# The second sequence's last two transforms over even and odd rows apart, and two waits of TensorE for its own last product, in a Fourier transform with two layers behind it

## The chip, the cores and the metric

The kernel runs on one core of a Trainium2 chip. The metric is the device time of one execution in microseconds; the profile gives the span from the first to the last instruction and every instruction's start and duration. The engines are TensorE (PE; its weight loads are listed apart as PEld), VectorE (DVE), ScalarE (ACT), GpSimd (POOL) and SyncE (SP), which issues most DMAs.

## The reference

```python
batch, seq, dim = (2, 3008, 256)        # x; d_ff = 2048
def _attn_ref(x):
    X = np.fft.fft(x, axis=1)
    X = np.fft.fft(X, axis=2)
    return X.real.astype(np.float32)
def _moe_ref(x, w_in, w_out):
    h = x @ w_in
    g = h * (1.0 / (1.0 + np.exp(-h)))
    return (g @ w_out).astype(np.float32)
def _moe2_ref(x, w_in, w_out, alpha):
    h = x @ w_in
    g = np.maximum(h, 0.0) + alpha * np.minimum(h, 0.0)
    return (g @ w_out).astype(np.float32)
# x -> _attn_ref -> reshape(6016, 256) -> _moe_ref -> _moe2_ref
```

The real part of a two-dimensional Fourier transform of two sequences is followed by two layers of 256 to 2048 to 256 features over all 6016 tokens.

## The kernel before, in words

**Transforms.** The feature transform is folded into the first layer's weights (`ab`). The transform over 3008 positions is folded by symmetry to 377 rows, held in three tiles of 128 (even rows in the first 192 places, odd rows in the last 192), and done with cosine tables for four blocks of output positions (`BLOCK_K`). Blocks 0 and 1 ("t1") already work on even and odd rows apart: one sum over the even rows (E), one over the odd rows (O), and the two blocks are E + O and E - O. Blocks 2 and 3 ("t2", "t3") are each one product over all three tiles, 376 or 378 columns wide, for each of the two halves p and q of the features (`transform23`, L571). These products are in float32, which TensorE does in two passes; the trace has a record for each pass. Everything else is split into high and low parts, and a product is three matmuls in fp32r of one pass each (`three`, L363 to L365).

**First layer.** It runs in `STEPS1` = 96 steps g: six chunks of 502 tokens by 16 slices of 128 hidden features. In step g TensorE does `first1(g)` (6 matmuls) and `second1(g - 2)` (12 matmuls, L626, L627 and L630). Between them ACT copies v out of PSUM (L927), DVE makes h in three operations (L1218, L1221, L1223), ACT makes the activation twice (L860 into `gh`, L863 into `g_sb`), and POOL subtracts them to `gl` (L1388), for which the last four matmuls of the step, L630, wait (`gl_done`).

**Turns.** The first sequence's transforms run before the steps. Those of the second run as jobs after certain steps (`JOB_AFTER`). A step or a job is a turn, and turns alternate between two pairs of PSUM banks; `turn_free` makes a turn wait until the turn before the last was read out. So while jobs stand between steps, each step waits for the h of the step just before it.

**The row of middle features.** Row 0 of the operands belongs to the middle feature. For block 3 of the second sequence it is made early, kept in `n_hold`, and written over row 0 of `pq` once the last t3 transform has been split: `n_hold_round` on ACT and `n_hold_low` on DVE (L1174), in step 38. SP waits for that (`t23_lo` at its full count), stores the rows of chunks 3 to 5 to DRAM (`store_n`, L437), waits for it, and loads chunk 3's row back over all partitions (`load_n(3)`, L431). POOL adds the two parts of what was loaded (`add_n`, L1326): `add_n(3)` stands behind `gl` of step 40, and POOL takes its work in program order:

```python
                if f == NF // 2 and c + 1 < NC1:
                    add_n(c + 1)
```

with `c, f = divmod(g, 16)`, and in it `pool.wait_ge(n_in, 16 * c)`.

**Second layer.** It has 48 units of 7 products of 3 matmuls (a fast scheme with seven products for eight, `products_a` and `products_b`) and 24 matmuls of `second2` (L684, L685, L688). Its weights are prepared by POOL and ACT during the steps from `W_STEP` on.

Of the kernel before, what the change touches and what calls it, by code (L numbers as in the profile page):

```python
# [7 lines left out]
F32 = mybir.dt.float32  # L8
# [4 lines left out]
P = 128  # L13
# [3 lines left out]
S2, S4, S8 = S // 2, S // 4, S // 8  # L17
QT = -(-(S8 + 1) // P)
NT = QT * BATCH
BLOCK_K = [list(range(1, S2, 4)), [S2 - k for k in range(1, S2, 4)], list(range(2, S2, 4)), list(range(0, S2 + 1, 4))]  # L20
BLOCK_W = [len(k) + len(k) % 2 for k in BLOCK_K]
BLOCK_AT = [sum(BLOCK_W[:i]) for i in range(4)]
COLS = sum(BLOCK_W)
# [15 lines left out]
A_JOBS = [(1, 0), (0, 0), (1, 1), (0, 1), (1, 2), (0, 2), (1, 3), (0, 3)]  # L39
FOLD_AFTER = [*range(3, 16, 2), *range(18, 32)]  # L40
IDLE = 4
JOB_AFTER = {1: "n", 33: "t1p", 34: "t1q", 35: "t2", 36: "t3"}


def cut(at, width):
# [20 lines left out]
def build(nc, x_tiles, x_half, moe_w_in, moe_w_out, moe2_w_in, moe2_w_out, alpha_cols, feat_dft, two_eye, t1, t2, t3, out_t):  # L66
    ctx = ExitStack()
    with ctx:
# [190 lines left out]
        def item_view(i):  # L259
# [5 lines left out]

        T_JOBS = [(1, 0, "p"), (1, 0, "q"), (2, 0, "p"), (2, 0, "q"), (3, 0, "p"), (3, 0, "q"), (3, None, "n"),
                  (1, 1, "p"), (1, 1, "q"), (2, 1, "p"), (2, 1, "q"), (3, 1, "p"), (3, 1, "q")]
        T1_JOBS = [j for j in T_JOBS if j[0] == 1]

        T23_JOBS = [j for j in T_JOBS if j[0] > 1] + ["n_hold"]  # L270

# [12 lines left out]
        def t1_of(*job):  # L284
            return T1_JOBS.index(job) + 1

        def t23_of(*job):
            return T23_JOBS.index(job) + 1
# [8 lines left out]
        def pair_at(turn):  # L297
            return 2 * (TURNS.index(turn) % 2)
# [6 lines left out]
        def t_bank(blk, b, s):  # L305

            if s == "n":
                return pair_at("n") + blk - 2
            if b == 0:
                return {1: 1, 2: 4, 3: 6}[blk] + (2 if blk == 1 else 1) * (s == "q")  # L310
            if blk == 1:
                return pair_at("t1" + s) + 1
            return pair_at(f"t{blk}") + (s == "q")

        def e_bank(b, s):
            return t_bank(1, b, s) - 1

        A2_BANK, N0_BANK = 7, 2

        def turn_free(pe, turn):  # L320

            i = TURNS.index(turn)
            if i < 2:
                pe.wait_ge(t1_sum, i + 1)
                pe.wait_ge(o_done, i + 1)
                return
            former = TURNS[i - 2]
            if former == "n":
                pe.wait_ge(t23_lo, t23_of(3, None, "n"))
            elif former in ("t1p", "t1q"):  # L330
                pe.wait_ge(t1_sum, t1_of(1, 1, former[2]))
                pe.wait_ge(o_done, t1_of(1, 1, former[2]))
            elif former in ("t2", "t3"):
                pe.wait_ge(t23_lo, t23_of(int(former[1]), 1, "q"))
            else:
                pe.wait_ge(h_done, former + 1)

# [5 lines left out]
                eng.wait_ge(mm1, STEPS1)  # L343


        W_STEP = [41, 57]
        W_SUMS = {"s1": ("a21", "a22"), "s3": ("a11", "a21"), "s2": ("s1", "a11"), "s4": ("a12", "s2")}
        W_STAGE = ["a11", "a12", "a22", "a21"]
        W_HI_AT = {"a11": 0, "a12": 0, "a22": 1, "s1": 2, "s3": 3, "s2": 4, "s4": 5}
# [42 lines left out]
        def _(sp):  # L392
# [77 lines left out]
            sp.wait_ge(stage_lo, WO2_ITEM)  # L470
            load_w7(0)
            store_x1(0)
            sp.wait_ge(t1_lo, len(T1_JOBS))
            sp.wait_ge(t1_late, len(T1_JOBS))
            sp.wait_ge(t23_lo, len(T23_JOBS))
            store_n(NC1 // 2, NC1)
            sp.wait_ge(n_out, 64)
# [37 lines left out]
        def _(pe):  # L515
# [45 lines left out]
            def transform23(blk, b, s, qs=range(QT)):  # L561

                sb, w = (t2_sb, BLOCK_W[2]) if blk == 2 else (t3_sb, BLOCK_W[3])
                half = 1 if s == "q" else 0
                dst = ps[0:72 if s == "n" else P, t_bank(blk, b, s), 0:w]
                for q in qs:
                    if s == "n":
                        st = nop[:, q:q + 72]
                    else:
                        st = op_b[QT * b + q][:, {2: (3, 0), 3: (1, 2)}[blk][half], :]  # L570
                    ins = pe.matmul(dst, st, sb[:, q, half * w:(half + 1) * w], start=q == 0, stop=q == QT - 1)  # L571
                if q == QT - 1:
                    ins.then_inc(t_pe, 1)

            def job(name):

                turn_free(pe, name)
                if name == "n":
                    pe.wait_ge(nop_ready, BATCH)
                    transform23(3, None, "n")  # L580
                elif name in ("t1p", "t1q"):
                    pe.wait_ge(fold, fold_at(NT - 1) + 7)
                    for blk in range(2):
                        for q in (blk, blk + 1):
                            transform1(1, name[2], blk, q)
                else:
                    pe.wait_ge(fold, fold_at(NT - 1) + FOLDS)
                    for s in "pq":
                        transform23(int(name[1]), 1, s)

            def first1(g):

# [133 lines left out]
            transform23(3, 0, "q")  # L726
            job(JOB_AFTER[LAG - 1])
            for g in range(LAG, STEPS1):
                first1(g)
                second1(g - LAG)  # L730
                if g in JOB_AFTER:
                    job(JOB_AFTER[g])
# [3 lines left out]
            second1(STEPS1 - 1)  # L736
            for u in range(1, UNITS):
                products_a(u)
                second2(u - 1, 0)
                second2(u - 1, 1)  # L740
                products_b(u)
                second2(u - 1, 2)
                second2(u - 1, 3)
# [5 lines left out]
        def _(act):  # L749
# [26 lines left out]
                act.wait_ge(fold, fold_rest_at(t) + 1)  # L776
                act.copy(op_b[t][:, 0, 0:1], nfold3[:, 3, NT + t:NT + t + 1]).then_inc(middle_in, 1)

            def t1_copy(b, s):

                act.wait_ge(t_pe, t_pe_of(1, b, s))
                if b:
                    act.wait_ge(t1_sum, 2)
                O = ps[:, t_bank(1, b, s), 0:T1W]
                if s == "q":
                    act.activation(o_sb[:, 2, :], O, ACT.Identity, scale=n_sign[:, 0:1])
                act.copy(o_sb[:, "pq".index(s), :], O).then_inc(o_done, 1)

            def t1_round(b, s):

# [11 lines left out]
            def t23_round(blk, b, s):  # L802

                act.wait_ge(t_pe, t_pe_of(blk, b, s))
                bank = t_bank(blk, b, s)
                if s == "n":
                    act.wait_ge(t23_lo, t23_of(blk, 0, "q"))
                    act.copy(n_hold[0:1, 0:BLOCK_W[blk]], ps[32:33, bank, 0:BLOCK_W[blk]])
                for c, o, a, w in cut(BLOCK_AT[blk], BLOCK_W[blk]):
                    if s == "n":  # L810
                        ins = act.copy(pq[0:1, c, 2, o:o + w], ps[0:1, bank, a:a + w])
                    else:
                        ins = act.copy(pq[:, 3 * b + c, 2 * (s == "q"), o:o + w], ps[:, bank, a:a + w])
                ins.then_inc(t23_hi, 1)

            def n_hold_round():
# [117 lines left out]
            for g in range(1, STEPS1):  # L934
                if g >= 2:
                    silu_high(g - 1)
                    copy_v(g)
                    silu_whole(g - 1)
                if g % NF == LAG - 1 and g >= NF:
                    store_x1_minus(g // NF - 1)  # L940
                if g == 1:
                    t23_round(3, 0, "p")
                    t23_round(3, 0, "q")
                turn = JOB_AFTER.get(g)
                if turn == "n":
                    t23_round(3, None, "n")
                elif turn in ("t1p", "t1q"):
                    t1_copy(1, turn[2])
                elif turn in ("t2", "t3"):
                    t23_round(int(turn[1]), 1, "p")  # L950
                    t23_round(int(turn[1]), 1, "q")
                former = JOB_AFTER.get(g - 1)
                if former in ("t1p", "t1q"):
                    t1_round(1, former[2])
                    t1_late_round(1, former[2])
                elif former == "t3":
                    n_hold_round()
                if 2 <= g <= 2 * WO2_ITEM - 4 and g % 2 == 0:
                    split_hi(g // 2 + 1)
                for q, at0 in enumerate(W_STEP):  # L960
                    for w, k in W_HI_AT.items():
                        if g == at0 + k:
                            w7_round(q, w)
                if g in X_STEP_HI:
                    xr_round(0, X_STEP_HI.index(g))
# [38 lines left out]
        def _(dve):  # L1004
# [124 lines left out]
            def t1_sums(b, s):  # L1129
# [9 lines left out]
                                                (ALU.add, ALU.subtract)[blk])  # L1139
                ins.then_inc(t1_sum, 1)  # L1140

            def t1_low(b, s):

                dve.wait_ge(t1_hi, t1_of(1, b, s))
                for blk, a, w, hi, raw, lo in t1_pieces(b, s, 0):
                    ins = dve.tensor_tensor(lo, raw, hi.bitcast(F32), ALU.subtract)
                ins.then_inc(t1_lo, 1)
# [62 lines left out]
            for g in range(STEPS1):  # L1210
# [23 lines left out]
                if turn == "n":  # L1234
                    t23_low(3, None, "n")
                elif turn in ("t1p", "t1q"):
                    t1_sums(1, turn[2])
                elif turn in ("t2", "t3"):
                    t23_low(int(turn[1]), 1, "p")
                    t23_low(int(turn[1]), 1, "q")  # L1240
                former = JOB_AFTER.get(g - 2)
                if former in ("t1p", "t1q"):
                    t1_low(1, former[2])
                    t1_late_low(1, former[2])
                elif former == "t3":
                    n_hold_low()
                if g in FOLD_AFTER:
                    i = FOLD_AFTER.index(g)
# [292 lines left out]
```

## Time and profile before

| what | value |
|---|---|
| median of 3 runs | 948.46 us |
| the three runs | 934.04, 948.46 and 949.15 us |
| the profiled execution | 928.23 us |
| its span, and mean granted clock | 926.3 us, 0.999 |
| PE, PEld busy | 920.9 us, 757.8 us |
| DVE, ACT, POOL busy | 625.9, 561.3 and 573.4 us |

Busy time of PE is modelled and overlaps from one matmul to the next (a matmul of 502 columns is listed with 385 ns, and the next starts 0.22 us after it), so pace is read from starts, not from durations.

### The profile page before, as it was taken

How to read it: one execution, taken by the hardware profiler on the slowest of the kernel's cores; microseconds unless marked ns; L12 is line 12 of the kernel's file. 1: busy time of each engine (PE TensorE's matmuls, PEld its weight loads, DVE VectorE, ACT ScalarE, POOL GpSimd, SP SyncE). 2: the span in 40 equal slices, each digit the busy share in tenths (PEclk: the TensorE clock that was granted, in tenths of full speed). 3: DMA queues.
4: the chain of work that ended last, by engine and by line, in shares of the span. 5: the costliest groups of instructions: out<-in, count | busy, mean ns of one | idle time of the engine just before them, and what ended most of it. 6: DMA issues, size and time to landing. Idle time of an engine off the chain costs nothing.

```text
span 926.3 us, 11845 instructions
## 1 busy us (share of the span) xinstructions
PE 920.9 (99%) x4034; PEld 757.8 (82%) x4034; DVE 625.9 (68%) x964; ACT 561.3 (61%) x873; POOL 573.4 (62%) x408
## 2 busy tenths in 40 slices
PE   9999999999999999999999999999999999999998
PEld 4688888778888888888888888888888888888886
DVE  5877799464544544544877777787787777777774
ACT  4677666557668666676765555565555555555554
POOL 0477655337877867676697477566647756764443
PEclk9999999999999999999999999999999999999999
DMA  9510200002110220100400200020020002001001
GB/s 354 231 56 24 90 1 1 1 1 90 45 46 23 70 66 1 45 1 1 136 1 1 90 1 1 1 89 1 1 90 1 0 1 90 1 1 44 1 1 45
DMA packets 19825, 40.35 MB, mean 44 GB/s; under 512 B 1802, under 2 KB 15668, under 8 KB 18740
## 3 DMA queue, kind: packets, MB, share of 16 engines
q1 hardware_dynamic: 18980, 39.05, 12.0%
q8 instruction: 32, 0.52, 0.2%
q10 hardware_dynamic: 688, 0.52, 0.2%
q14 instruction: 29, 0.24, 0.1%
q0 software_dynamic: 96, 0.02, 0.0%
HBM read 27.22 MB, written 12.37 MB: 43 GB/s over the span
## 4 chain that ended last, share of the span: by engine, by line
PE 99%; ACT 0%; DVE 0%; issue 0%
PE ps L363 13%; PE ps L365 13%; PE ps L364 13%; PE ps L626 9%; PE ps L630 9%; PE ps L627 9%; PE ps L688 9%; PE ps L684 9%; PE ps L685 9%; PE ps L571 2%; PE ps L527 2%; PE ps L556 1%; PE ps L552 1%; PE ps L694 0%; PE ps L543 0%; ACT out_sb L998 0%
## 5 line engine op out<-in xcount | busy, mean ns | idle before, releaser
L1410 POOL TENSOR_TENSOR gl<-g,gh 128x502 fp32r<-128x502 f32 x192 | 224.8, 1177 | 173.4 <-ACT gh L906 173.3
L1388 POOL TENSOR_TENSOR gl<-g_sb,gh 128x1004 fp32r<-128x1004 f32 x96 | 207.9, 2165 | 134.2 <-ACT g_sb L863 133.8
L900 ACT ACTIVATE g<-ps 128x502 f32<-128x502 f32 x192 | 112.0, 592 | 109.8 <-DVE ps L1267 104.9
L1218 DVE SCALAR_TENSOR_TENSOR h_sb<-n_all,a,ps 128x502 f32<-128x502 f32 x96 | 70.7, 736 | 140.9 <-ACT v_sb L927 140.6
L860 ACT ACTIVATE gh<-h_sb 128x1004 fp32r<-128x1004 f32 x96 | 100.6, 1048 | 90.1 <-DVE h_sb L1223 90.1
L1274 DVE SCALAR_TENSOR_TENSOR g<-g,less_alpha,ps 128x502 f32<-128x502 f32 x192 | 132.7, 732 | 32.7 <-ACT g L900 32.7
L626 PE MATMUL ps<-gh,wo 128*128 128x502 f32 x384 | 148.6, 387 | 0.0
L627 PE MATMUL ps<-gh,wo 128*128 128x502 f32 x384 | 147.4, 384 | 0.0
L685 PE MATMUL ps<-gh,wo 128*128 128x502 f32 x382 | 147.2, 385 | 0.0
L684 PE MATMUL ps<-gh,wo 128*128 128x502 f32 x382 | 147.2, 385 | 0.0
L906 ACT CAST gh<-g 128x502 fp32r<-128x502 f32 x192 | 113.0, 614 | 40.3 <-DVE g L1274 38.6
L688 PE MATMUL ps<-gl,wo 128*128 128x502 f32 x382 | 116.3, 385 | 0.0
L1267 DVE TENSOR_TENSOR ps<-ps,h 128x502 f32<-128x502 f32 x144 | 98.1, 689 | 5.0
L630 PE MATMUL ps<-gl,wo 128*128 128x502 f32 x384 | 101.4, 385 | 0.0
L863 ACT ACTIVATE g_sb<-h_sb 128x1004 f32<-128x1004 f32 x96 | 100.7, 1049 | 0.0
L626 PEld LDWEIGHTS ps<-gh,wo 128*128 128x128 f32 x384 | 72.0, 187 | 14.4
L630 PEld LDWEIGHTS ps<-gl,wo 128*128 128x128 f32 x384 | 72.0, 188 | 13.7
L688 PEld LDWEIGHTS ps<-gl,wo 128*128 128x128 f32 x382 | 71.7, 188 | 13.7
L684 PEld LDWEIGHTS ps<-gh,wo 128*128 128x128 f32 x382 | 71.7, 188 | 13.6
L685 PEld LDWEIGHTS ps<-gh,wo 128*128 128x128 f32 x382 | 71.7, 188 | 13.6
L627 PEld LDWEIGHTS ps<-gh,wo 128*128 128x128 f32 x384 | 72.1, 188 | 13.1
L363 PE MATMUL ps<-pq,ab 128*128 128x502 f32 x192 | 75.9, 396 | 0.0
(137 smaller groups left out, 1583.0 us busy)
## 6 DMA issues: line engine op xcount, KB each, us to landing
x_tile<-x_tiles SPq DMA_DIRECT2D x6, 1024.0 KB, 13.4
x_rows<-x SPq DMA_DIRECT2D x6, 1004.0 KB, 5.9
out_t<-out_sb SPq DMA_DIRECT2D x11, 502.0 KB, 3.2
x_raw_b<-x_rows SPq DMA_DIRECT2D x18, 251.0 KB, 4.2
stage<-moe_w_out SPq DMA_DIRECT2D x16, 256.0 KB, 4.1
n_parts<-n_rows SPq DMA_DIRECT2D x5, 502.0 KB, 3.5
stage<-moe_w_in SPq DMA_DIRECT2D x8, 256.0 KB, 3.5
w_sb<-moe_w_in SPq DMA_DIRECT2D x3, 512.0 KB, 8.7
```

The source lines that it names most:

```text
L363: pe.matmul(dst, sh, mh, start=first, stop=False)
L364: pe.matmul(dst, sh, ml, start=False, stop=False)
L365: return pe.matmul(dst, sl, mh, start=False, stop=last)
L626: pe.matmul(dst, wh, gh[g % 2][:, sg, :], start=f == 0, stop=False)
L627: pe.matmul(dst, wl, gh[g % 2][:, sg, :], start=False, stop=False)
L630: ins = pe.matmul(dst, wo1[:, f, 0, ft * P:(ft + 1) * P], gl[g % 2][:, sg, :], start=False, stop=f == NF - 1)
L684: pe.matmul(out[ft], wh, gh4[:, k, :], start=fp == 0 and k < 2, stop=False)
L685: pe.matmul(out[ft], wl, gh4[:, k, :], start=False, stop=False)
L688: ins = pe.matmul(out[ft], wo2[:, f, 0, ft * P:(ft + 1) * P], gl4[:, k, :], start=False, stop=fp == HF - 1 and k >= 2)
L1274: dve.scalar_tensor_tensor(out=g4[:, k, :], in0=g4[:, k, :], scalar=less_alpha[:, f:f + 1], in1=product_bank(u, TILE_IN[k]), op0=ALU.mult, ...
L1388: pool.tensor_tensor(gl[g % 2][:, :, :], g_sb[g % 2][:, :, :], gh[g % 2][:, :, :].bitcast(F32), ALU.subtract).then_inc(gl_done, 1)
L1410: pool.tensor_tensor(gl4[:, k, :], g4[:, k, :], gh4[:, k, :].bitcast(F32), ALU.subtract).then_inc(gl_done, 1)
```

## The change

The columns of blocks 2 and 3 are put in another order: first the positions k up to a quarter of the sequence, then their mirror images. For the mirror image of k the even rows count alike and the odd rows with the other sign, so `transform23_parted` makes E and O with half the columns (188 or 189) each, from four matmuls of 128, 64, 64 and 128 rows. ACT copies O to SBUF, DVE makes E + O and E - O, ACT rounds them and DVE makes the low parts (`t23_sums`, `t23_parted_round`, `t23_parted_low`). Each half p and q is now a turn by itself, so there are six jobs instead of four, after steps 32 to 37. The work on `n_hold` stands three and four steps behind the last job, where it stood one and two steps behind; in steps that is 40 (ACT) and 41 (DVE). The second layer's weights are prepared two steps later. TensorE waits for the end of `second1(0)` ahead of `first1(3)`, and for the end of its last product ahead of the first `second2` of the second unit.

```diff
-BLOCK_K = [list(range(1, S2, 4)), [S2 - k for k in range(1, S2, 4)], list(range(2, S2, 4)), list(range(0, S2 + 1, 4))]
+BLOCK_K = [list(range(1, S2, 4)), [S2 - k for k in range(1, S2, 4)], [*range(2, S4, 4), *(S2 - k for k in range(2, S4, 4))],
+           [*range(0, S4 + 1, 4), *(S2 - k for k in range(0, S4, 4))]]
...
-JOB_AFTER = {1: "n", 33: "t1p", 34: "t1q", 35: "t2", 36: "t3"}
+JOB_AFTER = {1: "n", 32: "t1p", 33: "t1q", 34: "t2p", 35: "t2q", 36: "t3p", 37: "t3q"}
...
-        W_STEP = [41, 57]
+        W_STEP = [43, 59]
...
+            def transform23_parted(blk, s):
+
+
+                sb, w = (t2_sb, BLOCK_W[2]) if blk == 2 else (t3_sb, BLOCK_W[3])
+                half, h = w * (s == "q"), w // 2
+                m = {2: (3, 0), 3: (1, 2)}[blk][s == "q"]
+                for o, parts in ((0, ((0, 0, P), (1, 0, P // 2))), (1, ((1, P // 2, P), (2, 0, P)))):
+                    dst = ps[:, e_bank(1, s, blk) + o, 0:h]
+                    for i, (q, r0, r1) in enumerate(parts):
+                        ins = pe.matmul(dst, op_b[QT + q][r0:r1, m, :], sb[r0:r1, q, half:half + h],
+                                        start=i == 0, stop=i == 1)
+                ins.then_inc(t_pe, 1)
...
-                    for s in "pq":
-                        transform23(int(name[1]), 1, s)
+                    transform23_parted(int(name[1]), name[2])
...
+                if g == LAG + 1:
+                    pe.wait_ge(mm2, 1)
                 first1(g)
...
                 products_a(u)
+
+                if u == 1:
+                    pe.wait_ge(prod_a, 8)
                 second2(u - 1, 0)
...
-                elif former == "t3":
+                elif former != "n":
+                    t23_parted_round(int(former[1]), former[2])
+                if JOB_AFTER.get(g - 3) == "t3q":
                     n_hold_round()
...
+            def t23_sums(blk, s):
+
+
+                dve.wait_ge(o_done, t1_of(blk, 1, s))
+                h, m = BLOCK_W[blk] // 2, 2 * (s == "q") + 1
+                for half in range(2):
+                    for c, o, a, w in cut(BLOCK_AT[blk] + half * h, h):
+                        E, O = ps[:, e_bank(1, s, blk), a:a + w], o_sb[:, "pq".index(s), a:a + w]
...
-                elif former == "t3":
+                elif former != "n":
+                    t23_parted_low(int(former[1]), former[2])
+                if JOB_AFTER.get(g - 4) == "t3q":
                     n_hold_low()
```

The first place is TensorE at the last transform job, with the end of `second1` ahead of it and the first matmul of the next step behind it; before:

```order
L630 MATMUL ps<-gl_92,wo_83 128x502 [waits gl_done]
L630 MATMUL ps<-gl_92,wo_83 128x502 x3
L571 MATMUL ps<-t_sb,op_b_58 128x378 [waits fold,t23_lo]
L571 MATMUL ps<-t_sb,op_b_59 128x378
L571 MATMUL ps<-t_sb,op_b_60 128x378
L571 MATMUL ps<-t_sb,op_b_58 128x378
L571 MATMUL ps<-t_sb,op_b_59 128x378
L571 MATMUL ps<-t_sb,op_b_60 128x378
L363 MATMUL ps<-pq,ab 128x502 [waits h_done]
```

And with the change, on the same engine at the same place:

```order
L641 MATMUL ps<-gl_93,wo_83 128x502 [waits gl_done]
L641 MATMUL ps<-gl_93,wo_83 128x502 x3
L583 MATMUL ps<-t_sb,op_b_58 128x189 [waits fold,o_done,t1_sum]
L583 MATMUL ps<-t_sb,op_b_59 128x189 x2
L583 MATMUL ps<-t_sb,op_b_60 128x189
L362 MATMUL ps<-pq,ab 128x502 [waits h_done]
```

A job of six matmuls of 378 columns has become two of four matmuls of 189 columns, with a step between them; the two in the middle, on `op_b_59`, take 64 rows each.

The second place is DVE from step 37 on: three operations L1218, L1221 and L1223 are the h of one step, and L1174 is the low part of the `n_hold` row, on which SP waits. Before, two steps' h and then it:

```order
L1218 SCALAR_TENSOR_TENSOR h_sb_79<-n_all_76,a_162,ps 128x502 [waits silu_done,v_done]
L1221 TENSOR_TENSOR h_sb_79<-ps,v_sb 128x502
L1223 TENSOR_TENSOR h_sb_79<-ps,h_sb_79 128x502 [waits w_done]
L1218 SCALAR_TENSOR_TENSOR h_sb_78<-n_all_76,a_162,ps 128x502 [waits silu_done,v_done]
L1221 TENSOR_TENSOR h_sb_78<-ps,v_sb 128x502
L1223 TENSOR_TENSOR h_sb_78<-ps,h_sb_78 128x502 [waits w_done]
L1174 TENSOR_TENSOR pq<-n_hold,pq 1x378 [waits t23_hi]
```

With the change the same row is L1221; ahead of it stand the last low parts of t3 (L1185, in steps 38 and 39) and the h of steps 39 to 41 (L1265, L1268 and L1270):

```order
L1185 TENSOR_TENSOR pq<-pq_raw,pq 128x378 [waits t23_hi]
L1265 SCALAR_TENSOR_TENSOR h_sb_79<-n_all_76,a_162,ps 128x502 [waits silu_done,v_done]
L1268 TENSOR_TENSOR h_sb_79<-ps,v_sb 128x502
L1270 TENSOR_TENSOR h_sb_79<-ps,h_sb_79 128x502 [waits w_done]
L1185 TENSOR_TENSOR pq<-pq_raw,pq 128x378 [waits t23_hi]
L1265 SCALAR_TENSOR_TENSOR h_sb_78<-n_all_76,a_162,ps 128x502 [waits silu_done,v_done]
L1268 TENSOR_TENSOR h_sb_78<-ps,v_sb 128x502
L1270 TENSOR_TENSOR h_sb_78<-ps,h_sb_78 128x502 [waits w_done]
L1265 SCALAR_TENSOR_TENSOR h_sb_79<-n_all_76,a_162,ps 128x502 [waits silu_done,v_done]
L1268 TENSOR_TENSOR h_sb_79<-ps,v_sb 128x502
L1270 TENSOR_TENSOR h_sb_79<-ps,h_sb_79 128x502 [waits w_done]
L1221 TENSOR_TENSOR pq<-n_hold,pq 1x378 [waits t23_hi]
```

The row has moved from step 38 to step 41.

The third place is POOL at step 40: L1388 is `gl` of one step, L1326 is `add_n(3)`, L1340 the first work on the second layer's weights. Before:

```order
L1388 TENSOR_TENSOR gl_92<-g_sb_81,gh_90 128x2x502 [waits silu_done,gh_done]
L1326 TENSOR_TENSOR n_all_76<-n_parts 128x502 [waits w_done,n_in]
L1388 TENSOR_TENSOR gl_93<-g_sb_82,gh_91 128x2x502 [waits silu_done,gh_done]
L1340 TENSOR_TENSOR w_raw_s_109<-stage_158,stage_157 128x512 [waits stage_in3,t_pe,stage_in2,t23_lo,stage_in1,stage_in0]
L1388 TENSOR_TENSOR gl_92<-g_sb_81,gh_90 128x2x502 [waits silu_done,gh_done]
```

With the change (`gl` is L1436, `add_n` L1374 and the weights L1388):

```order
L1436 TENSOR_TENSOR gl_92<-g_sb_81,gh_90 128x2x502 [waits silu_done,gh_done]
L1374 TENSOR_TENSOR n_all_76<-n_parts 128x502 [waits w_done,n_in]
L1436 TENSOR_TENSOR gl_93<-g_sb_82,gh_91 128x2x502 [waits silu_done,gh_done]
L1436 TENSOR_TENSOR gl_92<-g_sb_81,gh_90 128x2x502 [waits silu_done,gh_done]
L1436 TENSOR_TENSOR gl_93<-g_sb_82,gh_91 128x2x502 [waits silu_done,gh_done]
L1388 TENSOR_TENSOR w_raw_s_109<-stage_158,stage_157 128x512 [waits stage_in3,t_pe,stage_in2,t23_lo,stage_in1,stage_in0]
```

The work on the weights has moved back by two steps; `add_n(3)` stands where it stood, behind `gl` of step 40.

## Rows read from the trace of the kernel before

**Rows 1.** The page's first part: busy time, share, instructions.

```profile
PE 920.9 (99%) x4034; PEld 757.8 (82%) x4034; DVE 625.9 (68%) x964; ACT 561.3 (61%) x873; POOL 573.4 (62%) x408
```

**Rows 2.** The waits of PE, whole run: total, times, longest (us).

```profile
PE ps L694 <- DVE pq_raw L1178: 1.2, 1, 1.2
```

**Rows 3.** The chain that ended last, steps 35 to 38: start, length (us), what.

```profile
184.55 0.89 PE ps L630 x4
185.44 3.79 PE ps L571 x12
...
192.37 0.89 PE ps L630 x4
193.26 3.81 PE ps L571 x12
...
200.21 0.89 PE ps L630 x4
...
204.23 0.89 PE ps L630 x4
```

**Rows 4.** The timeline of PEld (weight loads), around a product of one row.

```profile
33.79 0.19 PEld L365 LDWEIGHTS ps<-pq,ab 128*128 128x128 f32 x1
34.33 0.29 PEld L543 LDWEIGHTS ps<-pq,ones 1*128 1x128 f32 x2 [0.36 <-issue]
34.98 0.19 PEld L363 LDWEIGHTS ps<-pq,ab 128*128 128x128 f32 x1 [0.36 <-issue]
35.09 0.19 PEld L364 LDWEIGHTS ps<-pq,ab 128*128 128x128 f32 x1
```

**Rows 5.** The timeline of PE at the same place.

```profile
34.01 0.39 PE L365 MATMUL ps<-pq,ab 128*128 128x502 f32 x1
34.33 0.72 PE L543 MATMUL ps<-pq,ones 1*128 1x502 f32 x2
```

**Rows 6.** The timeline of PE, in steps 36 and 38.

```profile
190.19 0.39 PE L365 MATMUL ps<-pq,ab 128*128 128x502 f32 x1
...
202.06 0.39 PE L365 MATMUL ps<-pq,ab 128*128 128x502 f32 x1
...
204.06 1.06 PE L630 MATMUL ps<-gl,wo 128*128 128x502 f32 x4
```

**Rows 7.** The timeline of ACT: v copied out, with a job and without one.

```profile
191.54 0.57 ACT L927 COPY v_sb<-ps 128x502 f32<-128x502 f32 x1
...
202.48 0.58 ACT L927 COPY v_sb<-ps 128x502 f32<-128x502 f32 x1 [0.24 <-PE ps L365]
```

**Rows 8.** The timeline of DVE: the last third of h, and the `n_hold` row.

```profile
193.40 0.67 DVE L1223 TENSOR_TENSOR h_sb<-ps,h_sb 128x502 f32<-128x502 f32 x1
...
204.34 0.67 DVE L1223 TENSOR_TENSOR h_sb<-ps,h_sb 128x502 f32<-128x502 f32 x1
204.92 1.79 DVE L1174 TENSOR_TENSOR pq<-n_hold,pq 1x378 fp32r<-1x378 f32 x1
```

**Rows 9.** The timeline of SP's queue after it.

```profile
206.80 1.39 SPq L437 DMA_DIRECT2D n_rows<-pq  x2
209.41 0.33 SPq L431 DMA_DIRECT2D n_parts<-n_rows  x1
```

**Rows 10.** L431's own view, its five loads.

```profile
DMA to landing us min/median/max: 3.4/3.5/4.2
```

**Rows 11.** The timeline of POOL, `gl` of steps 40 and 41.

```profile
216.21 2.16 POOL L1388 TENSOR_TENSOR gl<-g_sb,gh 128x1004 fp32r<-128x1004 f32 x1 [1.85 <-ACT g_sb L863]
218.32 1.08 POOL L1326 TENSOR_TENSOR n_all<-n_parts 128x502 f32<-128x502 f32 x1
220.22 2.17 POOL L1388 TENSOR_TENSOR gl<-g_sb,gh 128x1004 fp32r<-128x1004 f32 x1 [0.82 <-ACT g_sb L863]
```

**Rows 12.** Stretches: start:end, length, PE busy to POOL busy, granted clock, DMA.

```profile
450.00:900.00 450.00, 450.00 (x2017) 378.02 (x2016) 335.59 (x499) 253.64 (x449) 284.06 (x241) 1.00 0.08 27
922.40:926.30 3.90, 0.00 (x0) 0.00 (x0) 0.00 (x0) 0.26 (x1) 0.00 (x0) 0.88 0.70 264
```

More of the change, by code:

```diff
@@ L267, in build @@
                   (1, 1, "p"), (1, 1, "q"), (2, 1, "p"), (2, 1, "q"), (3, 1, "p"), (3, 1, "q")]
-        T1_JOBS = [j for j in T_JOBS if j[0] == 1]
+        T1_JOBS = [j for j in T_JOBS if j[0] == 1 or j[1] == 1]
         T23_JOBS = [j for j in T_JOBS if j[0] > 1] + ["n_hold"]
@@ L310, in t_bank, with e_bank @@
                 return {1: 1, 2: 4, 3: 6}[blk] + (2 if blk == 1 else 1) * (s == "q")
[L311 to L316, printed above, removed]
+            return pair_at(f"t{blk}{s}") + 1
+        def e_bank(b, s, blk=1):
+            return t_bank(blk, b, s) - 1
         A2_BANK, N0_BANK = 7, 2
@@ L329, in turn_free @@
                 pe.wait_ge(t23_lo, t23_of(3, None, "n"))
[L330 to L334, printed above, removed]
+            elif isinstance(former, str):
+                pe.wait_ge(t1_sum, t1_of(int(former[1]), 1, former[2]))
+                pe.wait_ge(o_done, t1_of(int(former[1]), 1, former[2]))
             else:
@@ L472, in _ @@
             store_x1(0)
[L473 to L474 removed]
+            sp.wait_ge(t1_lo, 2 * BATCH)
+            sp.wait_ge(t1_late, 2 * BATCH)
             sp.wait_ge(t23_lo, len(T23_JOBS))
@@ L777, in middle2, with t1_copy @@
                 act.copy(op_b[t][:, 0, 0:1], nfold3[:, 3, NT + t:NT + t + 1]).then_inc(middle_in, 1)
-            def t1_copy(b, s):
-                act.wait_ge(t_pe, t_pe_of(1, b, s))
+            def t1_copy(b, s, blk=1):
+                act.wait_ge(t_pe, t_pe_of(blk, b, s))
                 if b:
-                    act.wait_ge(t1_sum, 2)
-                O = ps[:, t_bank(1, b, s), 0:T1W]
-                if s == "q":
+                    act.wait_ge(t1_sum, t1_of(blk, b, s) - 2)
+                w = BLOCK_W[blk] // (1 if blk == 1 else 2)
+                O = ps[:, t_bank(blk, b, s), 0:w]
+                if s == "q" and blk == 1:
                     act.activation(o_sb[:, 2, :], O, ACT.Identity, scale=n_sign[:, 0:1])
-                act.copy(o_sb[:, "pq".index(s), :], O).then_inc(o_done, 1)
+                act.copy(o_sb[:, "pq".index(s), 0:w], O).then_inc(o_done, 1)
             def t1_round(b, s):
@@ L813, in t23_round, with t23_parted_round @@
                         ins = act.copy(pq[:, 3 * b + c, 2 * (s == "q"), o:o + w], ps[:, bank, a:a + w])
+                ins.then_inc(t23_hi, 1)
+            def t23_parted_round(blk, s):
+                act.wait_ge(t1_sum, t1_of(blk, 1, s))
+                for c, o, a, w in cut(BLOCK_AT[blk], BLOCK_W[blk]):
+                    m = 2 * (s == "q")
+                    ins = act.copy(pq[:, 3 + c, m, o:o + w], pq_raw[:, 3 + c, m + 1, o:o + w])
                 ins.then_inc(t23_hi, 1)
@@ L946, in _ @@
                     t23_round(3, None, "n")
[L947 to L952, printed above, removed]
+                elif turn:
+                    t1_copy(1, turn[2], int(turn[1]))
+                former = JOB_AFTER.get(g - 1, "n")
                 if former in ("t1p", "t1q"):
@@ L1140, in t1_sums, with t23_parted_low @@
                 ins.then_inc(t1_sum, 1)
+            def t23_sums(blk, s):
[4 more added lines that the diff above has]
+                        E, O = ps[:, e_bank(1, s, blk), a:a + w], o_sb[:, "pq".index(s), a:a + w]
+                        if half and (blk, s) == (3, "q"):
+                            E, O = O, E
+                        ins = dve.tensor_tensor(pq_raw[:, 3 + c, m, o:o + w], E, O, (ALU.add, ALU.subtract)[half])
+                ins.then_inc(t1_sum, 1)
+            def t23_parted_low(blk, s):
+                dve.wait_ge(t23_hi, t23_of(blk, 1, s))
+                for c, o, a, w in cut(BLOCK_AT[blk], BLOCK_W[blk]):
+                    m = 2 * (s == "q")
+                    ins = dve.tensor_tensor(pq[:, 3 + c, m + 1, o:o + w], pq_raw[:, 3 + c, m + 1, o:o + w],
+                                            pq[:, 3 + c, m, o:o + w].bitcast(F32), ALU.subtract)
+                ins.then_inc(t23_lo, 1)
             def t1_low(b, s):
@@ L1237, in _ @@
                     t1_sums(1, turn[2])
[L1238 to L1241, printed above, removed]
+                elif turn:
+                    t23_sums(int(turn[1]), turn[2])
+                former = JOB_AFTER.get(g - 2, "n")
                 if former in ("t1p", "t1q"):
```

## The prediction

> **What bounds the kernel now.** Read the page's first part and then the waits. PE is busy for 99% of the span and no other engine for more than 68% [rows 1]; in the whole run PE is listed as waiting once, 1.2 us at the very start [rows 2]. The chain that ended last is PE from one end to the other, so its places tell what a step costs: from one group of L630 to the next without a job 4.02 us (200.21 to 204.23), for 18 matmuls, 223.3 ns each; with a transform job in between 7.82 us (184.55 to 192.37) [rows 3]. So the kernel is a string of 3888 matmuls of 502 columns (96 steps of 18, 48 units of 45; 868 us) with the transforms and the start around it. Only two sorts of edit can move the end: work taken out of that string, and a gap put into it. Anything on DVE, ACT, POOL or a queue counts only when it comes late for PE.
>
> **The level of a run.** The profiled execution took 928.23 us, its span 926.3, so 1.9 us lie around it. The three timed ones took 934.04, 948.46 and 949.15. The trace shows no place where 20 us could be found but the string itself: 20.2 us over 3888 matmuls is 5.2 ns each, 228.5 ns instead of 223.3. I make the sum against 928.23 and treat the level as a question of its own below.
>
> **Part 1, the transforms.** Before, each of two jobs is 12 passes of 376 or 378 columns in 3.79 and 3.81 us, 316 ns a pass, 7.6 us together [rows 3]. After, four turns have 8 passes each of 188 or 189 columns. 316 ns is 378 columns at 0.84 ns; by that, a pass of 188 takes 158 ns, a turn 1.27 us, four 5.1 us. But the middle matmuls use 64 rows. The nearest thing in the trace is L543, a product over one row: its weight load is not made ahead but starts 0.32 us after L365's start, at 34.33, and weight loads stand 0.11 us apart (34.98 and 35.09), so its product starts near 34.44, 0.43 us behind L365 instead of 0.22 [rows 4, 5]; on the way back the load of L363 stands at 34.98, again 0.32 us behind the second L543. A change between whole and partial rows so costs 0.21 us, and a turn has two: 1.7 us, four 6.8 us, a gain of **0.8 us**. Ends: two such changes and a third between the halves, 1.9 us a turn, no gain; none, and the two halves beside each other, 0.95 us a turn, gain 3.8. I take 0.8, as the rows of L543 are the same event.
>
> The Trainium skill, "TensorE: Matmul & The Clock Gate" (Part 3), says that matmuls on different row groups run at the same time; the halves stand on rows 0 to 63 and 64 to 127, and by it the sum would be up to 1.3 us lower. No row here shows two such products side by side, so it moves only my lower end.
>
> **Part 2, turns that share a pair of banks.** From step 33 to 38 each step needs the h of the step just before. In step 36 of before, with ACT busy with earlier rounds, h was done (193.40 + 0.67) 3.9 us after v's last product started at 190.19; v's copy began only at 191.54, while without jobs it begins 0.42 us after that product's start (202.06, 202.48) [rows 6 to 8]. After, PE has 0.22 + 12 x 0.223 + 1.3 to 1.9, so 4.2 to 4.8 us of its own work there. The cover holds by 0.3 us or more: **0**, upper end 1.5 us if ACT's additional rounds delay v by another 0.6 us in five steps.
>
> **Part 3, the row in n_hold.** This is the term that I put most on. DVE's L1174 moves from step 38 to step 41, and behind it hang SP's store, SP's load and, on POOL, `add_n(3)`, which stays in step 40 with everything that POOL has to do queued behind it. In the times of before: L1174 starts at 204.92 and ends at 206.71 [rows 8]; SP issues the store at 206.80 and, when that has landed, the load at 209.41 [rows 9]; it lands 3.4 to 4.2 us later [rows 10], at 213.6 at the latest. POOL asks for it at 218.32, so 4.7 us are to spare [rows 11]. Three steps later, 12.06 us: L1174 ends at 218.77, the load is issued at 221.47 and lands at 225.7 (4.2 us; I take the long one, as a 1 MB store is issued right behind it). POOL stands from 218.4 to 225.7. Then L1326 takes 1.08 and `gl` of step 41 2.17 us: done at 228.9, where before it ended at 222.39 [rows 11]. PE asks for it with L630 at 204.06 + 5 x 4.02 = 224.16 [rows 3, 6]. With 0.1 us for the weight load [rows 4] L630 starts at 229.1: a gap of **4.9 us** in the string. Then POOL, with 2.17 us of `gl` in a step of 4.02 and the weights' work put back two steps, has caught up a step later, so it is paid once. Lower end 2.9: landing after 3.4 us, and L1174 in 0.6 instead of 1.79 us (a like third of h takes 0.67 over 128 rows [rows 8]). Upper end 5.5, a store slower by 0.6. The threshold is plain: up to 7.2 us of delay are free (4.7 of the landing, the 0.82 that POOL idles ahead of `gl` at 220.22, 1.8 between `gl` and L630), and 12.06 are asked for.
>
> **Part 4, PE's waits for its own last product.** A product's result is taken by another engine when its listed 0.39 us are over plus 0.03 (202.06, 202.48) [rows 6, 7]; then come semaphore and weight load, 0.11 [rows 4]: 0.53 us from start to start in place of 0.22, so **0.3 us** each, 0.6 together. Ends: 0.21, as for L543, and 0.45 if the load's whole 0.19 us has to pass. Queued behind each wait is PE's own string; the others lose nothing, since their idle time is larger in every step (ACT waits 0.24 us for v alone in a step without a job [rows 7]).
>
> **The sum.** 928.23 - 0.8 + 0 + 4.9 + 0.6 = 932.9 us; with all lower ends 928.23 - 3.8 + 2.9 + 0.4 = 927.7, with all upper ends 928.23 + 0 + 1.5 + 5.5 + 0.9 = 936.1.
>
> **Rivals.**
>
> *The string stays at the slow level.* If timed runs of the changed kernel keep the 228.5 ns a matmul that 948.46 implies, the gap is added to the median instead: 948.46 + 4.7 = 953 us, slower than before. It turns on the pace: above 227.3 ns a matmul the changed kernel is above 948.46. For it: two of three runs stood there, nothing in the profile says what sets it, and steps 2 to 95 pass six jobs that restart the string anyway, as before. Against it: both new waits empty PE at the start of each stage, and the gap of part 3 restarts it once more; if the level is a matter of how the string starts, they can set it. 0.3.
>
> *The gap isn't there* (the row is not late, because SP's chain is quicker than in the trace, or POOL's order differs from what is built): 928.23 - 0.8 + 0.6 = 928.0 us. It needs the chain of 6.9 us (206.71 to 213.6) to shrink to 2.0. 0.08 with the low level.
>
> *The transforms gain nothing and the turns stall:* 936 us, in the range of my forecast.
>
> *The clock falls in the gap.* Behind the last matmul the granted clock of the last 3.9 us is 0.88 [rows 12], which at 1.0 and 0.5 means that it fell from 2.4 to 1.2 GHz some 3 us after PE stopped. A gap of 4.9 us is longer. If it falls in the gap and stays low for a time as long as it took to fall, 3 us of matmuls take double: 1.5 us more, 934.5 us. 0.25 of all, inside the range. "TensorE: Matmul & The Clock Gate" of the Trainium skill (Part 1) names the same two levels and says that idleness brings the lower one; the trace agrees by the 0.88.
>
> *The waits themselves bring a pace quicker than 223.3.* No row shows one: the steps of the first stage stand 4.02 us apart [rows 3], and 450 us of the second hold 2017 matmuls [rows 12], 223.1 ns each. 0.02.
>
> **How the numbers follow.** Low level with the gap (clock steady or not): 0.55, 928 to 936, forecast **933 us**. High level: 0.33 (with the gap 0.3), around 953. No gap, low level: 0.08. Others 0.04. Both signs hold much, so the likeliest case's own range is 929 to 937; the range to be given must reach into the high level: **928 to 954**. Against the median of 948.46, 2% is about what a measurement of this kernel can tell from no change; faster by over 2% is below 929.5: the case without the gap, the low end of the forecast (mostly the transforms at their best), and a before that is measured higher: 0.17. Slower by over 2% needs the high level against a before that comes out near 934: 0.08. Within 2%: 0.75.
>
> **What would show it.** Right: on PE a wait on POOL's `gl` (L641) of 4 to 5 us in step 43, once, and on POOL `n_all` (L1374) waiting 7 us for the DMA of `n_parts`; L583 in four groups of 8 passes, 1.7 us each with weight loads not ahead in the middle; gaps of 0.3 us at the first L362 of step 3 and the first L695 of the second unit; no wait of PE between steps 32 and 38. Wrong: no wait of PE on POOL, or one that comes again in later steps; the L583 groups under 1.3 or over 1.9 us; above all, a pace other than 223.3 ns in the windows of the two stages, or timed runs that scatter as those of before did.

## The result, and the profile after

The changed kernel took 934.06 us, the median of 22 runs (932.76 to 935.58). The kernel before, run beside it 22 times, took 931.94 us (927.66 to 949.78). The ratio is 1.0044 with a 95% interval of 1.003 to 1.0058, for which the runs of before at 948 us and more are left out: the change costs 0.4%, and against the ten runs of before at 928 us alone (median 927.94) 0.7%. With all 22 runs in, the mean of before is 935.9 us and that of the changed kernel 934.0, so what the change costs depends on how often a run of before stands high. The forecast of 933 us was met within 1.1 us as a time; as a step from the median shown then (948.46) it had the wrong sign. Seven of the 22 runs of before stood at 948 to 950 us, four near 934 and the others mostly near 928; of the changed kernel none left its 3 us. That is a second effect of the change, and half of the experiments are about it.

The profiled execution took 933.65 us with a span of 931.8, 5.5 us more than before. PE's waits in the changed kernel (total, times, longest), to read beside [rows 2]:

```profile
PE ps L641 <- POOL gl L1436: 4.6, 1, 4.6
PE ps L705 <- DVE pq_raw L1225: 1.2, 1, 1.2
PE ps L526 <- DMA mt<-feat_dft: 0.5, 1, 0.5
```

The first line is new, and it is a single wait; the third, new too, is for a load at the start. The timeline of POOL shows what was ahead of it, to read beside [rows 11]:

```profile
214.84 2.17 POOL L1436 TENSOR_TENSOR gl<-g_sb,gh 128x1004 fp32r<-128x1004 f32 x1 [1.85 <-ACT g_sb L889]
224.33 1.07 POOL L1374 TENSOR_TENSOR n_all<-n_parts 128x502 f32<-128x502 f32 x1 [7.32 <-DMA n_parts<-n_rows]
225.36 4.25 POOL L1436 TENSOR_TENSOR gl<-g_sb,gh 128x1004 fp32r<-128x1004 f32 x2
```

POOL stands idle for 7.32 us until the row of chunk 3 has landed; then come `add_n(3)` and two `gl` in a row. DVE's `n_hold` row and SP's queue behind it, beside [rows 8, 9]:

```profile
215.63 1.78 DVE L1221 TENSOR_TENSOR pq<-n_hold,pq 1x378 fp32r<-1x378 f32 x1
```

```profile
217.50 1.39 SPq L436 DMA_DIRECT2D n_rows<-pq  x2
220.10 0.33 SPq L430 DMA_DIRECT2D n_parts<-n_rows  x1
```

From the row's end at 217.41 to the load's issue are 2.69 us, and 4.2 more to POOL's start at 224.33: the same chain as before, begun three steps later. PE at the gap, its timeline:

```profile
222.58 0.39 PE L638 MATMUL ps<-gh,wo 128*128 128x502 f32 x1
227.55 1.47 PE L641 MATMUL ps<-gl,wo 128*128 128x502 f32 x4 [4.57 <-POOL gl L1436]
228.82 0.62 PE L362 MATMUL ps<-pq,ab 128*128 128x502 f32 x1
229.24 0.62 PE L363 MATMUL ps<-pq,ab 128*128 128x502 f32 x1
```

From 222.58 to 227.55 are 4.97 us in place of 0.22. And then the matmuls of the next step start 0.42 us apart, not 0.22. The stretches around it (length, busy of PE, PEld, DVE, ACT, POOL, granted clock, DMA):

```profile
224.00:226.00 2.00, 0.00 (x0) 0.00 (x0) 0.00 (x0) 0.00 (x0) 1.67 (x2) 1.00 0.92 345
226.00:228.00 2.00, 0.45 (x2) 0.41 (x3) 0.00 (x0) 0.00 (x0) 2.00 (x2) 1.00 0.68 147
228.00:229.00 1.00, 1.00 (x5) 0.78 (x4) 0.00 (x0) 0.00 (x0) 1.00 (x1) 0.63 0.66 237
229.00:230.00 1.00, 1.00 (x4) 0.81 (x3) 0.00 (x0) 0.89 (x1) 0.62 (x1) 0.50 0.03 12
230.00:231.00 1.00, 1.00 (x4) 0.76 (x3) 0.00 (x0) 0.15 (x1) 0.00 (x0) 0.50 0.00 0
231.00:232.00 1.00, 1.00 (x5) 0.81 (x4) 0.00 (x0) 0.43 (x1) 0.00 (x0) 0.66 0.00 0
```

By the shares of these stretches the granted clock is 0.50 from about 228.3 to 231.7: 1.2 in place of 2.4 GHz. PE had been empty for 4.6 us and was running again for 0.7 us when it fell. Eight matmuls take 0.2 us more each, 1.6 us. The Trainium skill's "TensorE: Matmul & The Clock Gate" (Part 1) has idleness bring this level, and the trace agrees: the fall comes behind the only long gap.

The chain at the last four turns, beside [rows 3]:

```profile
181.15 0.89 PE ps L641 x4
182.04 1.35 PE ps L583 x8
186.71 0.89 PE ps L641 x4
187.60 1.35 PE ps L583 x8
192.09 0.89 PE ps L641 x4
192.99 1.36 PE ps L583 x8
197.48 0.89 PE ps L641 x4
198.37 1.36 PE ps L583 x8
202.87 0.89 PE ps L641 x4
```

The steps are 5.56, 5.38, 5.39 and 5.39 us, against 4.02 without a job: four turns cost 5.6 us in place of 7.6, a gain of 2.0. The weight loads of the first turn:

```profile
181.66 0.41 PEld L583 LDWEIGHTS ps<-t_sb,op_b 128*128 128x128 f32 x2
182.29 0.30 PEld L583 LDWEIGHTS ps<-t_sb,op_b 64*128 64x128 f32 x4 [0.22 <-issue]
182.81 0.30 PEld L583 LDWEIGHTS ps<-t_sb,op_b 128*128 128x128 f32 x2 [0.22 <-issue]
183.31 0.19 PEld L362 LDWEIGHTS ps<-pq,ab 128*128 128x128 f32 x1 [0.20 <-DVE h_sb L1270]
```

Four loads of 64 rows fit into 0.30 us, where two of 128 take 0.30 too: lower and upper half are loaded side by side. The loads that aren't made ahead, by 0.22 us at each change of mode, are there as well. The last row is a wait for h, 0.2 us, once.

The two waits for its own product, the timeline of PE:

```profile
44.42 1.05 PE L641 MATMUL ps<-gl,wo 128*128 128x502 f32 x4
45.54 0.49 PE L362 MATMUL ps<-pq,ab 128*128 128x502 f32 x1
45.87 0.39 PE L363 MATMUL ps<-pq,ab 128*128 128x502 f32 x1
...
451.74 0.38 PE L364 MATMUL ps<-x_t,w_s 128*128 128x502 f32 x1
452.18 0.49 PE L695 MATMUL ps<-gh,wo 128*128 128x502 f32 x1
452.51 0.39 PE L696 MATMUL ps<-gh,wo 128*128 128x502 f32 x1
```

At each, two starts are 0.44 and 0.33 us apart instead of twice 0.22 (451.74, 452.18, 452.51): 0.33 us, two 0.65. PE also comes to step 2 later than before: its L641 stands at 44.42, before L630 stood at 44.12, 0.3 us that the transforms and the waits have no part in. The wait for h is in the 5.6 us of the turns. So the sum of what the trace shows is -2.0 + 4.75 + 1.6 + 0.65 + 0.3 = 5.3 of the 5.5 us.

### The profile page after: what moved, and what is told of

It reads as the page before. It is cut to its first block, busy times and chain, and to the rows that moved or that the text cites. A ratio compares the mean times of both kernels' runs of the same rounds, so it can differ in the third digit from the quotient of the medians.

```text
span 931.8 us, 11884 instructions
## 1 busy us (share of the span) xinstructions
PE 921.0 (99%) x4042; PEld 757.4 (81%) x4042; DVE 630.9 (68%) x974; ACT 562.1 (60%) x877; POOL 573.7 (62%) x408
## 4 chain that ended last, share of the span: by engine, by line
PE 98%; issue 1%; POOL 0%; DMA 0%; ACT 0%; POOLq 0%
PE ps L362 13%; PE ps L364 13%; PE ps L363 13%; PE ps L695 9%; PE ps L696 9%; PE ps L699 9%; PE ps L641 9%; PE ps L637 9%; PE ps L638 9%; PE ps L526 2%; PE ps L555 1%; PE ps L570 1%; PE ps L583 1%; PE ps L551 1%; POOL gl L1436 0%
## 5 line engine op out<-in xcount | busy, mean ns | idle before, releaser
L1436 POOL TENSOR_TENSOR gl<-g_sb,gh 128x1004 fp32r<-128x1004 f32 x96 | 207.8, 2165 | 131.6 <-ACT g_sb L889 131.3
L1265 DVE SCALAR_TENSOR_TENSOR h_sb<-n_all,a,ps 128x502 f32<-128x502 f32 x96 | 70.7, 737 | 141.4 <-ACT v_sb L953 141.1
L641 PE MATMUL ps<-gl,wo 128*128 128x502 f32 x384 | 101.7, 387 | 4.6 <-POOL gl L1436 4.6
L641 PEld LDWEIGHTS ps<-gl,wo 128*128 128x128 f32 x384 | 72.0, 188 | 18.7 <-POOL gl L1436 5.0
```

The lines of the kernel that those rows point to most:

```text
L641: ins = pe.matmul(dst, wo1[:, f, 0, ft * P:(ft + 1) * P], gl[g % 2][:, sg, :], start=False, stop=f == NF - 1)
L1436: pool.tensor_tensor(gl[g % 2][:, :, :], g_sb[g % 2][:, :, :], gh[g % 2][:, :, :].bitcast(F32), ALU.subtract).then_inc(gl_done, 1)
```

## The experiments

**The gap, taken out.** In `addn42` the changed kernel's `add_n(3)` stands two steps later.

```diff
-                if f == NF // 2 and c + 1 < NC1:
+                if f == (10 if c == 2 else NF // 2) and c + 1 < NC1:
                     add_n(c + 1)
```

> The changed kernel with one condition altered: add_n(3) stands behind gl of step 42 on GpSimd instead of step 40, when the row is in by the times of the changed trace. My theory: the wait of PE on POOL's gl (4.7 us) goes, and with it the slow clock behind it (8 matmuls at 419 instead of 223 ns, 1.6 us): 934.1 - 6.3 = 927.7 us, and no wait of PE on POOL in the trace, granted clock 1.00 throughout. Rival: the row's chain only meets the next thing in POOL's order, and PE still waits: 932 or more. On the level: if the two waits of PE keep the string at its quick pace, none of the timed runs is near 947; if it was the long gap or the slow clock that did so, some are, as in the kernel before (7 of 22 at 948 to 950).

Measured: 926.65 us, the median of 12 runs (926.00 to 927.90), ratio to before 0.9971 (0.9953 to 0.9988). PE's waits hold only the one at the start:

```profile
PE ps L705 <- DVE pq_raw L1225: 1.2, 1, 1.2
```

and POOL no longer stands idle ahead of `add_n`:

```profile
222.54 2.17 POOL L1436 TENSOR_TENSOR gl<-g_sb,gh 128x1004 fp32r<-128x1004 f32 x1 [1.85 <-ACT g_sb L889]
224.66 1.08 POOL L1374 TENSOR_TENSOR n_all<-n_parts 128x502 f32<-128x502 f32 x1
```

The row's lateness, the gap and the slow clock were one thing, worth 7.4 us between the two medians (the two were not run side by side), where 6.3 were expected. This version beats both kernels. Against `before_waits` below, run beside it, which has the same two waits and whole transforms, it is 1.9 us quicker (926.65 and 928.59): what the parted transforms are worth by themselves.

**The gap, alone.** `before_hold41` is the kernel before with the late row.

```diff
-        W_STEP = [41, 57]
+        W_STEP = [43, 59]
...
-                elif former == "t3":
+                if JOB_AFTER.get(g - 4) == "t3":
                     n_hold_round()
...
-                elif former == "t3":
+                if JOB_AFTER.get(g - 5) == "t3":
                     n_hold_low()
```

> The kernel before with only the n_hold row's work in step 40 (ScalarE) and 41 (VectorE) instead of 37 and 38, and the second layer's weights two steps later, as in the change. Theory: PE waits once for POOL's gl by 4.7 to 4.9 us in step 43, then some 8 matmuls at half clock, 1.6 us: 928.2 + 6.4 = 934.6 us at the quick pace. Rival, that the gap comes from the parted transforms' own work on VectorE and ScalarE: no gap, 928. On the level: if a gap in the string in step 43 is what keeps the runs off 949, none is there; if not, they scatter as before does, moved up by 6 us.

Measured: 935.23 us in 5 runs (934.44 to 936.62), before 928.45 beside it. The wait is there without any parted transform, and the low clock lasted longer than in the changed kernel:

```profile
PE ps L630 <- POOL gl L1388: 4.6, 1, 4.6
```

```profile
226.00:227.00 1.00, 0.00 (x0) 0.00 (x0) 0.00 (x0) 0.00 (x0) 1.00 (x2) 0.78 0.38 127
228.00:229.00 1.00, 0.80 (x2) 0.72 (x3) 0.00 (x0) 0.00 (x0) 1.00 (x2) 0.50 0.97 261
229.00:233.00 4.00, 4.00 (x11) 3.14 (x11) 0.00 (x0) 1.26 (x2) 1.24 (x1) 0.50 0.09 35
```

Here the clock fell in the gap itself, at about 226.6 (a mean of 0.78 from 226 to 227), 1.6 us before PE ran again at 228.20, and was back at about 233.4. So 6.8 us against 6.4 expected: the same gap, and 12 matmuls at half clock, 2.5 us. Five runs are too few to say whether a gap alone steadies the level.

**The halves beside each other.** In `halves_apart`, made from `addn42`, the two products of 64 rows are separated by one of 128.

```diff
-                for o, parts in ((0, ((0, 0, P), (1, 0, P // 2))), (1, ((1, P // 2, P), (2, 0, P)))):
+                for o, parts in ((0, ((0, 0, P), (1, 0, P // 2))), (1, ((2, 0, P), (1, P // 2, P)))):
```

> As addn42 (926.65 us), with the order of the four matmuls of a parted transform changed from whole, lower half, upper half, whole to whole, lower half, whole, upper half, so that the two products of 64 rows no longer stand side by side. In the changed trace the two halves start 6 or 7 ns apart, and a turn costs 1.36 us. If running beside each other is what makes the turn short, it now costs two passes (0.16 us each) and two changes of mode (0.1 us each) more, 1.9 us, and the time is 2.0 us longer, 928.7. If it was the mode changes being cheap, the time stays within 0.8 us.

Measured: 929.25 us in 10 runs (928.59 to 930.00). Its chain at two of the turns:

```profile
186.32 0.89 PE ps L641 x4
187.21 1.86 PE ps L583 x8
192.40 0.89 PE ps L641 x4
```

A step with a turn takes 6.08 us instead of 5.38, so the order alone is worth 0.7 us a turn: two passes of 0.16 us that no longer run beside others, and two more changes of mode at 0.2, where 0.1 was expected. Against `addn42` the median is 2.6 us longer, where 2.0 were expected. Of the change's gain of 2.0 us in the transforms, all rests on this order: with the halves apart a turn costs 2.06 us, four 8.2, more than the 7.6 of whole transforms.

**The two waits, left out and put in alone.** `addn42_nowaits` is `addn42` without them; `before_waits` is the kernel before with nothing but them.

```diff
-                if g == LAG + 1:
-                    pe.wait_ge(mm2, 1)
...
-                if u == 1:
-                    pe.wait_ge(prod_a, 8)
```

> As addn42, and the two waits of PE for its own last product are left out too. Sum: 927.7 - 0.65 = 927.1 us where the string is at its quick pace. If the waits set the pace, runs at some 933 and 948 us come back here (about a third of the runs); if the shorter, parted transforms or their six turns set it, all runs stay within 1 us of 927.

Measured: 12 runs, seven from 925.69 to 927.60 and the others at 931.53, 947.04, 947.09, 947.78 and 952.60 us; median 927.58. The median of the seven is 926.63; with 5.4 us, 21.3 us and both added (the distances of the two levels from 928) it is 932.0, 947.9 and 953.3, and the five stand within 0.9 us of these. So the two levels come each by itself, and can add up.

```diff
+                if g == LAG + 1:
+                    pe.wait_ge(mm2, 1)
                 first1(g)
...
+                if u == 1:
+                    pe.wait_ge(prod_a, 8)
                 second2(u - 1, 0)
```

> The kernel before with nothing but the two waits of PE for its own last product. Theory that the waits set the pace: every run at 928.2 + 0.65 = 928.9 us, none at 934 or 949. Rival that they are mere gaps: the scatter of before (928, 934, 949) moved up by 0.65 us. As time alone they cost 0.65 us, read from two gaps of 440 and 331 ns each in place of 223 in the changed trace.

Measured: 928.59 us, 12 runs from 928.10 to 929.53, ratio 0.9996 (0.9982 to 1.001). Beside these the kernel before had 29 runs: 22 from 927.47 to 930.03, five near 933.6 and two near 949.9. Over all comparisons of this study it had 103: 20 at 933 to 936 and 12 at 948 to 950. The kernels with both waits (the changed one, `addn42`, `before_waits`, `halves_apart`) had 56, none of them up. It is the waits that steady the time, not the parted transforms, and not the gap, which three of the four don't have.

**One wait at a time.** `before_wait_step3` and `before_wait_unit1` have the first or the second of the two pieces above alone.

> The kernel before with the first of PE's two waits alone (ahead of step 3). If the 934 level (5.5 us, about 1080 matmuls at 5.2 ns, so one stage's worth) and the 949 level (both stages) are set by how the string starts in each stage, this wait takes away the part that the first stage gives, and runs at about 928.5 and, if the second stage can go slow by itself, 939 to 940 remain. If a slow pace is set once at the start and kept through the kernel, this wait alone makes all runs 928.5. If only the second wait matters, the scatter stays: 928, 934, 949.

Measured: 12 runs, ten from 928.03 to 930.62 and two at 949.65 and 949.85 us. Nothing near 934. The one at 930.62 is the profiled one: PE waited 1.0 us for a load at the start and came to L630 of step 2 at 46.25 in place of 44.12, and its pace was the quick one.

> The kernel before with the second of PE's two waits alone (in the second unit of the second layer). If each stage's pace is set where it starts, the first stage's slow part remains, 5 to 9 us (933 to 938), and none is at 949. If the pace is set once at the start and kept, the wait resets it from there on: the same times. If it does nothing alone: 928, 934, 949 as before.

Measured: 12 runs, eleven from 927.81 to 929.62 and one at 933.71. Nothing at 949. Each wait so seems to remove one level. Twelve runs each are few: at the rates of before (20 and 12 of 103), one set of twelve in 13 would have none at 934 by luck, and one in four none at 949. The next pair says more.

**The waits in other places.** `before_wait_unit24` has one wait, in the middle of the second layer; `before_wait_step18` has one, in the middle of the stretch from step 3 to the first transform job.

```diff
+                if u == 24:
+                    pe.wait_ge(prod_a, 4 * 25)
                 second2(u - 1, 0)
```

> The kernel before with one wait of PE for its own last product, in unit 24 of the second layer instead of unit 1. Theory: the 949 level is the second layer's whole string at some 233 instead of 223.3 ns a matmul (2160 x 9.7 ns = 21 us), and emptying PE ends it; so runs at 949 are gone and the same share of runs stands half way, near 928.6 + 10.3 = 939, while the 934 level stays. Rival: the wait acts only where the string starts (or the level has another cause, such as the loads of the second stage): 949 stays.

Measured: 12 runs, nine from 928.33 to 930.58, one at 934.21, and two at 938.46 and 938.86. None at 949. Both stand 0.6 us or less from the 939 expected, at a place where no run of any other kernel stood.

```diff
+                if g == 18:
+                    pe.wait_ge(mm2, 16)
                 first1(g)
```

> The kernel before with one wait of PE for its own last product, ahead of step 18 instead of step 3. Theory: the 934 level is the stretch from step 2 to the first transform job behind step 33 at 233 instead of 223.3 ns (some 560 matmuls x 9.7 ns = 5.4 us), which the job's restart ends; then a wait at half way leaves half of it: runs near 931.3 in place of 934, and 949 stays. Rival (a slow pace of 3.2 ns more over all of the first layer): the jobs don't end it, and runs stand near 929.5.

Measured: 12 runs, nine from 927.70 to 929.54, two at 931.02 and 931.09 where 931.3 was expected, and one of 5343 us, whose cause is not known and which tells nothing of the kernel. The profiled execution is the one at 931.02. Its chain across the wait:

```profile
98.71 0.93 PE ps L630 x4
102.91 0.93 PE ps L630 x4
107.11 0.95 PE ps L630 x4
115.53 0.89 PE ps L630 x4
123.57 0.89 PE ps L630 x4
```

and two stretches of it:

```profile
50.00:100.00 50.00, 50.00 (x216) 1.00 0.14 44
120.00:170.00 50.00, 50.00 (x225) 1.00 0.00 1
```

Up to step 18 a step takes 4.20 us, 233.3 ns a matmul; behind the wait it takes 4.02, 223.3 ns (115.53 to 123.57 are two steps). The granted clock is 1.00 in both, and PE waits for nothing. From 44.11 to 107.11 the slow steps stand without a change. The same trace shows where the slow pace began, at the job "n" after step 1, whose float32 passes end at 40.39:

```profile
36.20 0.39 PE L363 MATMUL ps<-pq,ab 128*128 128x502 f32 x1
36.42 0.39 PE L364 MATMUL ps<-pq,ab 128*128 128x502 f32 x1
40.91 0.40 PE L364 MATMUL ps<-pq,ab 128*128 128x502 f32 x1
41.15 0.40 PE L365 MATMUL ps<-pq,ab 128*128 128x502 f32 x1
```

Ahead of the job two starts are 0.22 us apart, behind it 0.24, and 0.23 from there on.

**Three looks at the kernel before.**

> The kernel before unaltered, one execution more with a profile, in the hope of one at 934 or 949 us (some three in ten are). If it is one: theory, that matmuls of 502 columns stand 228 to 229 ns apart instead of 223.3, over both stages at 949 and over part of one at 934, without a wait of PE; rival, that the time is lost in gaps or in the first 35 us of loads.

> The kernel before unaltered, one more execution with a profile. Only one at 934 or 949 tells anything: theory, steps of 4.19 us (18 x 233 ns) instead of 4.02 up to step 33 in a run at 934, units of 10.5 us instead of 10.05 in one at 949; rival, gaps.

> The kernel before unaltered, a third look, with the same expectations: in a run at 934, steps of 4.19 instead of 4.02 us up to step 33; in one at 949, units of 10.5 instead of 10.05 us; rival, gaps in the string or a longer start.

Measured: 928.26, 928.75 and 928.98 us. None fell on a higher level, so they tell nothing; the second layer at its slow pace has not been seen in a trace.

## Why the prediction was right in its time and wrong in its step

- **What bounds it.** Right: PE's string, in which only work and gaps count.
- **The reference.** Wrong, and the step that failed. I set the changed kernel's low level against 948.46 as where the kernel before stands, from three runs of which two were high, and so forecast 933 as a gain of 1.6%. Of 103 runs 12 stood there, and beside the changed kernel the median of before was 931.94. From the 928.23 us of the profiled execution my own sum was a loss of 4.7 us, and the two profiled executions are 5.4 us apart (928.23 and 933.65; by the ratio of the runs below 948 it is 4.1): the sum was made from the right number, the step from the wrong one.
- **The level's mechanism.** Half right. That the string's pace sets it was right, but not as one pace of 228.5 ns over all 3888 matmuls. It is 233.3 ns in one stretch: about 560 matmuls of the first layer by 10 ns give 5.6 us (measured 5.4 between levels), the 2160 of the second 21.6 (measured 21.3). That the slow pace of the first layer begins behind the job "n" and ends when PE is emptied is shown in one trace; that it otherwise ends at the first transform job is worked out from the 5.4 us, and no trace shows it. The second layer's rests on the 939 us of the wait in unit 24. I gave the rival of a lasting slow level 0.33; with both waits in, it was gone. Its argument that six jobs restart the string "as before" had the number wrong (before, there are four), and a job does not keep the string quick, as that trace shows.
- **Part 3, the row in `n_hold`.** Right in place, step and size: POOL idle 7.3 us for the DMA, one wait of PE in step 43, 4.75 us longer than the usual start to start; forecast 4.9.
- **The clock in the gap.** Its price was right (1.5 forecast, 1.6 measured, but 2.5 in `before_hold41`), its chance of 0.25 was too low: every run of the changed kernel has a mean granted clock of 0.996 to 0.998, those of `addn42` 0.999 or more. And it did not fall in the gap, as I had it, but 0.7 us behind it; in `before_hold41` it fell in the gap. It belonged in the sum, which would then have been 934.4.
- **Part 1, the transforms.** Right in direction, off in size: 0.8 us forecast, 2.0 measured. The changes of mode cost what L543 showed, 0.2 us; the two halves run beside each other, which I had left to the lower end, and the 1.3 us that I gave there for it are the difference. The Trainium skill's rule on row groups ("TensorE: Matmul & The Clock Gate", Part 3) holds here, and `halves_apart` shows it.
- **Part 2, turns on one pair of banks.** 0 forecast, 0.2 us once, within the turns' 5.6.
- **Part 4, the waits.** 0.6 forecast, 0.65 measured; what they do beyond that I held possible and no more.
- **No gap, 928 us.** It didn't come; that such a kernel gives 926.65 us was shown only by moving `add_n`.

## What to carry to other kernels

When a step is moved back, follow each thing that waits for it to the engine that takes it in program order: the row of one partition moved three steps, its reader on POOL stayed, and all of POOL's work stood behind it. A few runs of a kernel may stand on different levels; look at their scatter before you take a median as its time, and look for a level as a pace that holds over a stretch. In this kernel products of half the rows paid only beside each other.

## What the runs showed of the hardware that I had not expected

- A string of fp32r matmuls of 502 columns with their weight loads runs at one of two steady paces, 223.3 or 233.3 ns a matmul, at the same granted clock, 1.00. It stays on one for hundreds of matmuls. In the trace of `before_wait_step18` it came out of a float32 job on the slow one. In the same trace emptying PE once (0.33 us) turned the slow one into the quick one, and in 56 runs of kernels that do so at the start of both stretches none was slow. In none of the 103 runs of before can the 59 steps between its last job and the second layer have been slow: that would be 10.6 us, and none stood near 939. Why the string falls on one or the other, why emptying PE has always ended on the quick one, and whether a pause that does not empty it would do the same, stays open; nothing here looks into PE.
- With one and the same wait of 4.6 us without a matmul, the granted clock fell to 0.50 in the changed kernel 0.7 us after the matmuls had started again, and in `before_hold41` 1.6 us before they did. It stayed there for 3.4 us in the one and 6.8 us in the other, and cost 1.6 and 2.5 us.
- Products on rows 0 to 63 and 64 to 127 run beside each other in float32 too: four weight loads of 64 rows take the 0.30 us of two of 128, and with the order changed in `halves_apart` a turn takes 0.7 us more.
